# Weighing values by attention with the values stationary, in halves of the array, and raw scores in halves of its rows

## The chip, the core and the metric

One NeuronCore of a Trainium2 chip runs the whole program. The metric is the device time of one execution in microseconds; the kernel before and the kernel after are compared by the median of their runs. The engines have names in the profile: PE is TensorE's matmul, PEld its weight load, DVE is VectorE, ACT is ScalarE, POOL is GpSimd, SP issues the DMAs. They run side by side and meet only at semaphores.

## The reference

Attention over 2 batches, 8 heads, 768 positions and 64 values per head, with a mask: a query sees the first `n_sink` = 4 keys and the last `window` = 128 keys up to itself. Two feed-forward layers follow, on 1536 tokens of 512 values, 2048 hidden.

```
scores = q k^T / sqrt(64), masked;  a = softmax(scores);  x = a v
x = relu(x W_in)^2 W_out                                (layer 1)
h = x W2_in;  g = P(h) / (Q(h) + 1e-6);  out = g W2_out (layer 2)
P = a0 + a1 h + a2 h^2 + a3 h^3,  Q = 1 + |b0||h| + |b1| h^2
```

## The kernel before, in words

The time has three parts: a front in which only attention runs, layer 1, and layer 2. Layer 1 has four blocks of 384 tokens (3 tiles of 128) and 16 steps (`i`) a block. A step is 12 matmuls of `first1` (weights stationary, `xT` moving, 384 columns, into `h_ps`), the square on ACT and DVE (`relu`, `square`, `hidden`), and 12 of `second1` into `y_ps`. Both split each f32 operand into a rounded high part and a low part and make three products of type fp32r. The attention of later blocks is put between them: `events` gives a share to the middle of `first1` and to the middle of `second1` of each step, an order written out by hand and followed by every engine.

Attention has 96 units, one for each head of each query tile of 128. Unit u is tile `qt = u // 8`, head `m = u % 8`, and `i = qt % 6` is the tile's place in its batch. The units 0 to 29 (`LEAD = 30`) run in the front. Slot s does, in this order on PE: `score(s)`, `turn_p(s - 2)`, `weigh(s - 3)`.

- `score` (L1177): the keys of two tiles of 128 and, from `i = 2`, 32 columns with the sink keys, so 128, 256 or 288 columns. For the first 8 groups of four units (`EARLY = 8`) it is a raw f32 matmul (L1196) over 128 rows, of which the 64 lower ones hold zeros in q. Later k and q are split on POOL (`split_kq`, L475) and it is two fp32r matmuls (L1200). k and q are stored twice for that, in rows 0 to 63 and 64 to 127.
- DVE adds the mask and takes the row's greatest value in one instruction (`scores`, L918, output `bnegs`, a ring of 4).
- ACT makes the exponential and its sum (`exp`, L650). It writes `bprobs[:, r, cols, m % 4]`: the four heads of a group are interleaved, so a column of one head lies 16 bytes from the next.
- `turn_p` (L1204) transposes one or two tiles of it, and once for four heads the 32 x 4 sink columns of the group (L1218).
- DVE (even units) or ACT (odd units) copies the result to `bpT` (`pT_part`, L930 and L642).
- `weigh` (L1222): `bpT` (128 x 128) is stationary and 64 columns of `bv` move, so that the output has queries on the partitions (L1233). Once for four heads one product of the sinks with 256 moving columns (L1240) is added; `bvs` is zero outside the head's own block.
- When a tile's eight units are weighed, DVE sums and inverts the row sums and multiplies (`finish`, L938, into `o_sb`), PE turns `o_sb` by four transposes (`tile_out`, L1252), ACT writes the high part of `xT` (L672) and DVE the low part (L966).

POOL splits the weights (`weight_high` L456, `weight_low` L461), 8 tiles early (`EARLY_W = 8`), after which ACT makes the high parts and waits for the eighth at the end of step 0. SP issues all loads in order (`load_weights`, `load_k`, `load_q`, `load_v`, `load_sinks`), each behind a semaphore that frees its buffer.

PSUM has eight banks: four of `y_ps`, two of `s_ps`, `h_ps` and `o_ps`. In the front scores and transposes of odd units use banks of `y_ps`; in layer 1 there is one bank for scores and one for transposes.

## Time and profile before

| | us |
|---|---|
| median of 3 runs | 674.43 (673.2 to 674.54) |
| the profiled execution | 672.72 |
| its span, first to last instruction | 670.9 |
| PE busy | 654.5 (98%) |
| PEld busy | 617.3 (92%) |
| DVE busy | 447.9 (67%) |
| ACT busy | 377.7 (56%) |
| POOL busy | 330.9 (49%) |

Read these as averages over stages with different limits. Matmuls overlap one another, so that their durations add up to more than the time they take; the distance between starts is what one costs. A raw f32 matmul stands in the trace as two weight loads and two MATMULs.

### The profile page before, as it was taken

Reading aid. Unit: us, or ns where it says so; the run is one execution under the profiler, and the core shown is the slowest. Engines: PE = TensorE matmul, PEld = TensorE weight load, DVE = VectorE, ACT = ScalarE, POOL = GpSimd, SP = SyncE. Lnnn points to the kernel's source line nnn. Section 1 sums busy time; section 2 is a strip of 40 time slices with the busy share of each in tenths; the row PEclk is TensorE's granted clock in tenths of the full one; section 3 lists DMA queues with packets and bytes.
Section 4 is the critical chain, followed back from the end, with each engine's and each line's share of the span. In section 5 each row is a group of like instructions: output and inputs, shape, how many; then the busy total and the mean of one; then the engine's idle time right before and its main releaser. Section 6 shows DMA issues by size and latency. Waiting matters only on the chain.

```text
span 670.9 us, 10181 instructions
## 1 busy us (share of the span) xinstructions
PE 654.5 (98%) x3714; PEld 617.3 (92%) x3714; DVE 447.9 (67%) x665; ACT 377.7 (56%) x804; POOL 330.9 (49%) x316
## 2 busy tenths in 40 slices
PE   7999999999999999999999998999999999999997
PEld 6889998999999999999999997889899999999995
DVE  6656564444344344343466679999899989998995
ACT  3755555334444354443322256677877787778874
POOL 3968573313242212300022337777777767776773
PEclk9999999999999999999999999999999999999999
DMA  7743241203311113100043430002100210001001
GB/s 248 258 146 119 97 162 40 64 1 121 93 40 40 40 40 134 40 9 1 20 125 124 127 110 0 1 1 95 48 1 0 95 48 0 1 1 48 1 0 53
DMA packets 28971, 43.49 MB, mean 65 GB/s; under 512 B 4080, under 2 KB 19440, under 8 KB 28400
## 3 DMA queue, kind: packets, MB, share of 16 engines
q1 hardware_dynamic: 28912, 42.74, 19.6%
q8 instruction: 32, 0.52, 0.3%
q14 instruction: 27, 0.22, 0.1%
HBM read 36.44 MB, written 6.29 MB: 64 GB/s over the span
## 4 chain that ended last, share of the span: by engine, by line
PE 77%; DVE 14%; ACT 3%; issue 3%; POOL 2%; DMA 1%; DVEq 0%; SPq 0%; ACTq 0%; POOLq 0%
PE h_ps L1146 22%; PE y_ps L1158 18%; PE y_ps L1384 15%; PE s_ps L1146 7%; PE o_ps L1233 4%; PE o_ps L1146 3%; DVE s_ps L879 3%; PE s_ps L1216 2%; PE s_ps L1200 2%; DVE o_ps L879 2%; DVE sq L842 2%; DVE p_buf L882 1%; DVE p_buf L873 1%; DVE h_ps L879 1%; DMA y_scratch<-xT 1%
## 5 line engine op out<-in xcount | busy, mean ns | idle before, releaser
L1146 PE MATMUL h_ps<-xT,weights 128*128 128x384 f32 x960 | 190.2, 340 | 0.7 <-ACT sq L594 0.7
L1146 PEld LDWEIGHTS h_ps<-xT,weights 128*128 128x128 f32 x960 | 167.4, 188 | 2.5 <-issue 1.0
L1158 PE MATMUL y_ps<-hid,weights 128*128 128x384 f32 x768 | 156.7, 344 | 0.0
L1384 PE MATMUL y_ps<-weights,hid 128*128 128x512 f32 x576 | 144.3, 395 | 2.3 <-POOL hid L561 1.0
L1158 PEld LDWEIGHTS y_ps<-hid,weights 128*128 128x128 f32 x768 | 134.5, 188 | 0.7 <-issue 0.2
L1384 PEld LDWEIGHTS y_ps<-weights,hid 128*128 128x128 f32 x576 | 107.2, 188 | 24.3 <-POOL hid L561 2.4
L656 ACT ACTIVATE bprobs<-bnegs,neg_max 128x288 f32<-128x288 f32 (+2 forms) x96 | 72.0, 759 | 67.2 <-DVE neg_max L925 66.8
L842 DVE TENSOR_TENSOR sq<-sq 128x384 f32<-128x384 f32 x64 | 45.4, 710 | 88.9 <-ACT sq L594 88.8
L561 POOL TENSOR_TENSOR hid<-p_buf,hid 128x384 fp32r<-128x384 f32 x63 | 64.8, 1028 | 40.0 <-ACT hid L762 39.6
L552 POOL TENSOR_TENSOR q_buf<-h_abs,q_buf 128x384 f32<-128x384 f32 x64 | 64.8, 1013 | 34.5 <-ACT q_buf L617 32.0
L879 DVE RECIPROCAL s_ps<-q_buf 128x384 f32<-128x384 f32 x31 | 79.4, 2561 | 3.2
L848 DVE TENSOR_TENSOR hid<-sq,hid 128x384 fp32r<-128x384 f32 x64 | 53.4, 835 | 37.8 <-ACT hid L599 37.8
L482 POOL TENSOR_SCALAR bq_hi<-q_raw 128x512 fp32r<-128x512 f32 x16 | 10.7, 668 | 136.6 <-DMA q_raw<-in_q_pack 115.2
L458 POOL TENSOR_SCALAR weights<-weights_raw 128x1024 fp32r<-128x1024 f32 x24 | 26.2, 1092 | 104.3 <-DMA weights_raw<-in_w_pack 104.1
L594 ACT ACTIVATE sq<-h_ps 128x384 f32<-128x384 f32 x64 | 31.4, 491 | 74.6 <-PE h_ps L1146 74.6
L1146 PE MATMUL s_ps<-xT,weights 128*128 128x384 f32 x384 | 72.5, 337 | 0.0
L1146 PEld LDWEIGHTS s_ps<-xT,weights 128*128 128x128 f32 x384 | 68.3, 188 | 2.5
L556 POOL TENSOR_TENSOR p_buf<-p_buf,h_sb 128x384 f32<-128x384 f32 x64 | 65.3, 1020 | 0.0
L599 ACT ACTIVATE hid<-sq 128x384 fp32r<-128x384 f32 x64 | 33.6, 524 | 51.4 <-DVE sq L842 51.4
L925 DVE CUSTOM_DVE_ANT_0 bnegs<-s_ps,band_bias 128x288 f32<-128x288 f32 (+2 forms) x81 | 34.3, 423 | 36.2 <-PE s_ps L1200 30.3
L762 ACT ACTIVATE hid<-p_buf 128x384 fp32r<-128x384 f32 x63 | 33.0, 524 | 28.9 <-DVE p_buf L882 27.6
L617 ACT ACTIVATE q_buf<-h_abs,abs_b 128x384 f32<-128x384 f32 x64 | 45.4, 709 | 2.1
(102 smaller groups left out, 940.4 us busy)
## 6 DMA issues: line engine op xcount, KB each, us to landing
weights_raw<-in_w_pack SPq DMA_DIRECT2D x32, 512.0 KB, 4.6
bk_raw<-in_k_pack SPq DMA_DIRECT2D x24, 256.0 KB, 3.3
q_raw<-in_q_pack SPq DMA_DIRECT2D x24, 256.0 KB, 3.4
bv<-in_v_pack SPq DMA_DIRECT2D x24, 128.0 KB, 2.0
y_scratch<-xT SPq DMA_DIRECT2D x2, 1536.0 KB, 6.1
xT<-y_scratch SPq DMA_DIRECT2D x2, 1536.0 KB, 7.2
out_y<-out_stage SPq DMA_DIRECT2D x3, 768.0 KB, 3.5
out_y<-out_stage SPq DMA_DIRECT2D x3, 256.0 KB, 2.9
```

The lines of the kernel that those rows point to most:

```text
L552: pool.tensor_tensor(q_buf[:, i % RING, :], h_abs[:, i % RING, :], q_buf[:, i % RING, :], ALU.mult).then_inc(qmul_ready, 1)
L556: pool.tensor_tensor(p_buf[:, i % RING, :], p_buf[:, i % RING, :], h_sb[:, i % RING, :], ALU.mult).then_inc(pmul_ready, 1)
L561: pool.tensor_tensor(hid2[:, i % RING, LO, :], p_buf[:, i % RING, :], hid2[:, i % RING, HI, :].bitcast(F32), ALU.subtract).then_inc(hid_re ...
L617: nc.scalar.activation(q_buf[:, i % RING, :], h_abs[:, i % RING, :], ACT.Identity, scale=abs_b[:, 1:2], bias=abs_b[:, 0:1]).then_inc(lin_r ...
L656: nc.scalar.activation(bprobs[:, u // GROUP % 2, cols, m % GROUP], bnegs[:, u % N_RING, cols], ACT.Exp, scale=-1.0, bias=neg_max[:, m:m + ...
L842: nc.vector.tensor_tensor(sq[:, i % 2, :], sq[:, i % 2, :], sq[:, i % 2, :], ALU.mult).then_inc(act1_ready, 1)
L848: nc.vector.tensor_tensor(hid[:, i % 2, LO, :], sq[:, i % 2, :], hid[:, i % 2, HI, :].bitcast(F32), ALU.subtract).then_inc(hid_ready, 1)
L879: nc.vector.reciprocal(h_banks[r], q_buf[:, r, :]).then_inc(qinv_ready, 1)
L925: nc.vector.tensor_tensor_reduce(out=bnegs[:, u % N_RING, cols], in0=score_bank(u)[:, cols], in1=band_bias[:, kind, cols], scale=-SCALE, s ...
L1146: ins = nc.tensor.matmul(bank, weights[:, i, wp, W_IN, t * P:(t + 1) * P], x, start=(t == 0 and n == 0), stop=(t == KC - 1 and n == 2))
L1158: ins = nc.tensor.matmul(y_ps[:, m, 0:NT], weights[:, i, wp, W_OUT, m * P:(m + 1) * P], hid[:, i % 2, gp, :], start=(i == 0 and n == 0), s ...
L1384: ins = nc.tensor.matmul(y_bank(turn, t), hid2[:, i % RING, gp, t * P:(t + 1) * P], weights[:, i, wp, W_OUT, :], start=(i == 0 and n == 0) ...
```

## The change

Attention is regrouped. The unit of work is a pair of heads (`p`), 48 in all, and weighing takes four heads at once (`g`, 24 groups). 15 pairs run in the front, which are the same 30 heads and tiles. A step "A" scores pair p and, for odd p, weighs group (p - 3) / 2; a step "B" transposes pair p - 1; "F" turns the inverse sums; "M", "X" and "L" multiply and split the output.

- Weighing: `bv[:, t, 64 columns]` is stationary and 128 columns of `bpT` move. The output has the head's 64 values on partitions: the even head of a pair on 0 to 63, the odd one on 64 to 127. The sink product is made for each head. The output is born turned, so instead of it the inverse sums are spread over 512 columns (DVE), turned (PE, four transposes), copied (ACT), and multiplied (DVE).
- Raw scores: q and k of the two heads of a pair lie in rows 0 to 63 and 64 to 127, and each head's matmul uses its half of the rows. No zeros and no copy are loaded for them. k and q for the split scores are loaded apart (`load_kd`, `load_qd`), from group 6 and 8.
- `bprobs` has one row after the other for the heads, so that exp writes contiguously. DVE packs the sink columns of four heads into `bsinks` before they are transposed.
- Each pair's transposes go to two banks, of which DVE copies the first and ACT the second.
- The `bnegs` ring has 3 places, `bpT` holds two pairs; `EARLY_W` is 6.

```diff
-    LEAD = 30
+    P_ALL = PAIRS * TILES
+    LEAD = 15
+    EARLY_W = 6
     EARLY = 8
-    EARLY_W = 8
-    P_RING = 3
-    N_RING = 4
+    N_RING = 3
...
-        bprobs = sb("bprobs", [P, 2, BAND, GROUP], F32, band)
-        bpT = sb("bpT", [P, P_RING, 3 * P], F32, band)
+        bprobs = sb("bprobs", [P, 2, GROUP, BAND], F32, band)
+        bsinks = sb("bsinks", [P, 2, GROUP, SINK_CAP], F32, band)
+        bpT = sb("bpT", [P, (2 * GROUP + 1) * P], F32, band)
...
+        def steps(first, last):
+            found = []
+            for p in range(first, last):
+                qt = p // PAIRS - 1
+                found.append(("A", p))
+                if p % PAIRS == 1 and qt >= 0:
+                    found.append(("M", qt))
+                    found.append(("X", qt))
+                    if qt >= QT and qt % QT == QT - 1:
+                        found.append(("L", qt))
+                if p <= P_ALL:
+                    found.append(("B", p))
+                if p % PAIRS == 1 and qt >= 0 and not (qt >= QT and qt % QT == QT - 1):
+                    found.append(("L", qt))
+                if p % PAIRS == 0 and qt >= 0:
+                    found.append(("F", qt))
+            return found
...
+                for k in range(4, EARLY):
                     load_k(k)
                     load_q(k)
...
+                    load_weights(0, k)
+                    if k < EARLY - 2:
+                        load_kd(k + 2)
+                    if k == EARLY - 2:
+                        load_qd(EARLY)
+                    if k == EARLY - 1:
+                        load_kd(EARLY)
+                    load_v(k)
+                load_kd(EARLY + 1)
+                load_qd(EARLY + 1)
...
+                for i in range(EARLY_W - 2):
                     weight_high(0, i)
                     weight_low(i)
+                    if i == 1:
+                        split_sinks(0)
+                split_k(EARLY - 2)
+                split_k(EARLY - 1)
                 split_kq(EARLY)
+                for i in range(EARLY_W - 2, EARLY_W):
+                    weight_high(0, i)
+                    weight_low(i)
                 split_kq(EARLY + 1)
...
-                    nc.scalar.activation(bprobs[:, u // GROUP % 2, cols, m % GROUP], bnegs[:, u % N_RING, cols],
+                    nc.scalar.activation(bprobs[:, u // GROUP % 2, m % GROUP, cols], bnegs[:, u % N_RING, cols],
                                          ACT.Exp, scale=-1.0, bias=neg_max[:, m:m + 1],
...
+                def pack_sinks(g):
...
+                    nc.vector.tensor_copy(bsinks[:, g % 2, :, :], bprobs[:, g % 2, :, 0:SINK_CAP]
+                                          ).then_inc(sinks_packed, 1)
...
+                    nc.vector.tensor_copy(inv_rows[:, :, :], row_inv[:, :].rearrange("p (h o) -> p h o", o=1
+                                          ).to_broadcast([P, H, D])).then_inc(inv_spread, 1)
+
+                def divide(qt):
+
+                    dve.wait_ge(inv_copied, qt + 1)
+                    dve.wait_ge(g_pv, 2 * (qt + 1))
+                    nc.vector.tensor_tensor(inv_cols[:, :], o_ps[:, :], inv_cols[:, :], ALU.mult).then_inc(o_read, 1)
...
+                    for hp in range(2):
+                        if k < EARLY:
+                            rows = slice(D * hp, D * hp + D)
+                            ins = nc.tensor.matmul(pair_bank(p, hp)[:, cols],
+                                                   bq[rows, k % 3, P * (c % 2):P * (c % 2) + P], bk[rows, c, cols],
+                                                   start=True, stop=True)
+                            continue
...
+                def weigh(g):
+                    qt, c, i = pair(2 * g)
+                    wait_turned_copies(pe, 2 * g + 1)
+                    pe.wait_ge(bv_loaded[g % 4], 16 * (g // 4 + 1))
+                    if c == 0 and qt >= 1:
+                        pe.wait_ge(o_read, qt)
+                    last = c + 1 == KC - 1
+                    tiles = 1 if i == 0 else 2
+                    for t in range(tiles):
+                        for cc in (c, c + 1):
+                            for hp in range(2):
+                                at = D * (2 * cc + hp)
+                                ins = nc.tensor.matmul(o_ps[D * hp:D * hp + D, cc * P:(cc + 1) * P],
+                                                       bv[:, t, at:at + D], bpT[:, turned_at(cc, hp) + t * P:turned_at(cc, hp) + (t + 1) * P],
+                                                       start=(cc == 0 and t == 0),
+                                                       stop=(i < 2 and last and cc > c and t == tiles - 1),
+                                                       skip_group_check=True)
+                    if i >= 2:
...
+                                ins = nc.tensor.matmul(o_ps[D * hp:D * hp + D, cc * P:(cc + 1) * P],
+                                                       bvs[:, at:at + D], bpT[:, 2 * GROUP * P:(2 * GROUP + 1) * P], start=False,
+                                                       stop=(last and cc > c), skip_group_check=True)
```

## Rows read from the trace of the kernel before

**Rows 1.** The page: the span, and the first line of the engine totals.
```profile
span 670.9 us, 10181 instructions
...
PE 654.5 (98%) x3714; PEld 617.3 (92%) x3714; DVE 447.9 (67%) x665; ACT 377.7 (56%) x804; POOL 330.9 (49%) x316
```

**Rows 2.** Busy time by stretch (start:end, length, each engine), and a wait.
```profile
0.00:44.50 44.50, 39.21 (x237) 33.56 (x238) 28.39 (x107) 26.48 (x77) 27.59 (x26) 1.00 0.74 235
44.50:320.00 275.50, 271.14 (x1714) 267.13 (x1714) 127.60 (x303) 124.19 (x290) 92.30 (x80) 1.00 0.20 65
...
402.00:671.00 269.00, 262.18 (x1298) 234.62 (x1297) 240.64 (x198) 200.69 (x387) 191.37 (x192) 1.00 0.07 25
...
PE h_ps L1135 <- POOL ident L453: 2.0, 1, 2.0
```

**Rows 3.** Timeline of PE, one slot in layer 1: start, us, engine, line, operation.
```profile
190.68 1.21 PE L1146 MATMUL h_ps<-xT,weights 128*128 128x384 f32 x6
191.72 0.29 PE L1200 MATMUL s_ps<-bkT,bq_hi 128*128 128x288 f32 x1
...
191.99 0.39 PE L1216 MATMUL s_ps<-ident,bprobs 128*128 128x128 f32 x2
192.21 0.56 PE L1233 MATMUL o_ps<-bv,bpT 128*128 128x64 f32 x4
192.58 1.30 PE L1146 MATMUL h_ps<-xT,weights 128*128 128x384 f32 x6
193.72 1.22 PE L1158 MATMUL y_ps<-hid,weights 128*128 128x384 f32 x6
```

**Rows 4.** Timeline of PE in the front.
```profile
38.83 0.39 PE L1216 MATMUL s_ps<-ident,bprobs 128*128 128x128 f32 x2
39.05 0.56 PE L1233 MATMUL y_ps<-bv,bpT 128*128 128x64 f32 x4
39.45 0.65 PE L1240 MATMUL y_ps<-bvs,bpT 128*128 128x256 f32 x2
39.94 0.65 PE L1196 MATMUL y_ps<-bk_raw,q_raw 128*128 128x288 f32 x2
40.42 0.39 PE L1216 MATMUL y_ps<-ident,bprobs 128*128 128x128 f32 x2
```

**Rows 5.** Groups by line, 44.5 to 320 us (count | busy us, mean ns), and weight loads.
```profile
L1233 PE MATMUL o_ps<-bv,bpT 128*128 128x64 f32 x262 | 37.1, 261 | 0.3 <-DVE o_sb L949 0.3
...
L1240 PE MATMUL o_ps<-bvs,bpT 128*128 128x256 f32 x28 | 9.1, 407 | 0.0
...
L1146 PEld LDWEIGHTS h_ps<-xT,weights 128*128 128x128 f32 x960 | 167.4, 188 | 2.5 <-issue 1.0
```

**Rows 6.** Groups by line of ACT, over the whole span.
```profile
L656 ACT ACTIVATE bprobs<-bnegs,neg_max 128x288 f32<-128x288 f32 x64 | 52.1, 818 | 45.0 <-DVE neg_max L925 44.8
L617 ACT ACTIVATE q_buf<-h_abs,abs_b 128x384 f32<-128x384 f32 x64 | 45.4, 709 | 2.1
...
L647 ACT ACTIVATE bpT<-s_ps 128x256 f32<-128x256 f32 x17 | 6.5, 380 | 9.6 <-PE s_ps L1216 9.6
```

**Rows 7.** A group of DVE; timeline of POOL and DVE from 12 us.
```profile
L925 DVE CUSTOM_DVE_ANT_0 bnegs<-s_ps,band_bias 128x288 f32<-128x288 f32 x57 | 25.8, 453 | 26.9 <-PE s_ps L1200 23.4 <-PE s_ps L1196 3.5
...
12.08 2.36 POOL L463 TENSOR_TENSOR weights<-weights_raw,weights 128x1024 fp32r<-128x1024 f32 x1
...
12.71 1.77 DVE L889 TENSOR_SCALAR band_bias<-sq 128x32 bf16<-128x32 f32 x1
```

**Rows 8.** DMA issues (count, KB each, us to landing); timeline of POOL from 52 us.
```profile
weights_raw<-in_w_pack SPq DMA_DIRECT2D x32, 512.0 KB, 4.6
bk_raw<-in_k_pack SPq DMA_DIRECT2D x24, 256.0 KB, 3.3
...
53.19 2.57 POOL L463 TENSOR_TENSOR weights<-weights_raw,weights 128x1024 fp32r<-128x1024 f32 x1
```

563 lines of the change are left out of this document (287 added, 276 removed).

## The prediction

> **What bounds the kernel now.** I read the engine totals first, then busy time by stage. TensorE is busy 654.5 of 670.9 us, so the next question is where its rows differ [rows 1]. There are three stretches. Until 44.5 us lies the front: 30 of the 96 units of attention, with layer 1 not yet begun. TensorE is busy 39.2 of 44.5 us there, and 2.0 of the idle 5.3 us pass before its first instruction [rows 2]. From 44.5 to 320 us, layer 1 has the other units between its matmuls and TensorE is busy 271.1 of 275.5. What comes after 402 us is layer 2, which the change leaves alone. The granted clock is 1.00 in each [rows 2], so I give the clock no term. The bound is TensorE's instruction stream in the first 320 us; time that another engine saves there counts only where TensorE waits for it.
>
> So each piece of attention has to be priced in TensorE time, and a duration is the wrong price, since matmuls are pipelined. I take distances between starts. Six dense matmuls start at 190.68 and the next instruction at 191.72: 0.173 us each, though the six last 1.21, so that one lasts 0.34. Between the starts 190.68 and 193.72 lie twelve dense matmuls (2.08 us) and one unit, so a unit of 288 columns costs 0.96 us: two scores 0.27 (191.72 to 191.99), two transposes 0.22, and the rest, 0.47, for four weighing instructions, 0.115 each [rows 3]. In the front a raw score instruction of 288 columns costs 0.24 (39.94 to 40.42, two), a transpose 0.11 (38.83 to 39.05, two), a weighing instruction of 64 columns 0.10 (39.05 to 39.45, four), a sink instruction of 256 columns 0.245 [rows 4]. A raw f32 matmul is two instructions, as the counts of two show. A raw 128-column one should then stream 0.24 x 128/288 = 0.107 us; a 64-column one would need 0.053 but costs twice that, so its 128-column weight load sets its pace.
>
> **The change, part by part.**
>
> 1. Weighing in layer 1 (18 groups of four heads). Today: 262 instructions at 0.115 and 28 sink instructions [rows 5] at 0.24 x 256/288 = 0.21: 30.1 + 6.0 = 36.1 us. After: one matmul per head and key tile, two instructions, 64 stationary and 128 moving columns. 16 groups have two tiles (16 instructions), 2 have one (8), and 14 groups add 8 for the sinks, since each head now needs its own sink product: 272 + 112 = 384. One after the other at 0.11 they take 42.2 us, which is 6.1 more than now. If the two column halves work side by side, the order in the code (both instructions of one head, then both of the next) lets only the second of one head run with the first of the next: n instructions take n/2 + 1 places. That is 16 x 9 + 2 x 5 + 14 x 4 = 210 places; each needs 0.107 for the stream, and two loads of 64 columns, as much as the one load that costs 0.115 now: 24.2 us, a gain of 11.9. No row has two matmuls side by side, so the bounds are +6.1 and -11.9. I take the overlap because the halves share neither stationary columns nor output partitions, and a load already runs beside a dense matmul in every dense row.
>
> 2. Going over to halves and back. Two crossings per group of weighing, 36 in layer 1; in the front five per two pairs, 37 in all. No row shows one. From below: nothing, as the goings between raw and rounded matmuls at 191.99 and 192.58 leave the unit at the sum of its parts. From above: the last matmul must end (1.21 less 1.04 = 0.17 us [rows 3]) and the first load be made afresh (0.19 [rows 5]): 0.36. I take 0.15, nearest to the first of the two: the pipeline empties, the load is hidden. Layer 1: +5.4 us (0 to +13).
> The Trainium skill ("TensorEngine Tiling (Array Packing)", Tiling Modes) says that going to another tiling mode drains TensorE, and this speaks against the change; it gives no time. Without that rule the sum would be 8 us lower; with a drain at the upper bound, 13 us higher.
>
> 3. Raw scores in row halves, in the front: pairs 4 to 7 of 256 columns, 8 to 14 of 288. Four instructions per pair take three places: 4 x 0.21 + 7 x 0.24 = -2.5 us with overlap, 0 without. Weighing in the front, 27 units: 8 with one tile and 19 with two, 92 x 0.10, and 4 x 0.245 = 10.2 us now; after, 96 instructions, 54 places of 0.11 = 5.9 (10.6 without overlap): -4.3. Crossings 37 x 0.15 = 5.6, of which I count half, since TensorE idles 3.3 us there anyway and a wait also empties the pipeline: +2.8.
>
> 4. Exp in a row. Now 0.82 us for 288 columns. A contiguous ACTIVATE with pointers for scale and bias takes 0.71 for 384 [rows 6], so 288 lie between 0.53 (by columns alone) and 0.71; I take 0.63. 96 x 0.19 = up to 18 us of ACT, but ACT is busy 124 of 275 us in layer 1 [rows 2], so worth 0 there. In the front it shortens a chain that would be late next: with a pair's two exps (1.0 to 1.2) and a copy (0.38 for 256 columns [rows 6]), ACT needs 1.5 to 1.7 us a pair beside TensorE's 2.3. The stationary loads of the probabilities become contiguous too; a transpose already costs its stream, 0.11 against 0.107, so 0.
>
> 5. DVE gets more. Per pair: two reads of scores (0.45 each) [rows 7] and a copy (0.4, as ACT's [rows 6]), 1.3 us; per tile now also a spread of the inverses over 512 columns (like a product of 512 from SBUF, up to 0.7) beside the 0.7 us of multiplication and 0.7 of splitting, and per two pairs a packing of sinks (about 0.25): 1.3 + 2.1/4 + 0.12 = 1.9 us a pair. That fits under 2.3. But the spread and the packing read and write SBUF alone, and such operations of DVE are held while POOL runs: the bias of 32 columns that began at 12.71 ended at 14.48, with POOL's 12.08 + 2.36 = 14.44 [rows 7]. POOL is busy 27.6 of 44.5 us in the front and nearly always from 11 to 40. Three packings hold up the transposes of their pair directly. Six new operations at about half of a 2.4 us operation in the worst case give 0 to 7 us; I take +3 in the front, and +1 for the first block of layer 1.
> The Trainium skill ("SBUF — State Buffer", Who interferes with whom) calls this an exclusive lock that the later comer waits out in full; the row of the bias agrees.
>
> 6. Loads and POOL. Early k and q are no longer stored twice: of 256 KB each [rows 8] half goes, 8 x 256 KB less, but four doubled parts (kd 6 to 8, qd 8) come in their place, each with its issue on SP's in-order queue ahead of a v. A group then brings 1.15 MB per 4.6 us, 250 GB/s beside the 235 of now [rows 2]; they land in 3.3 to 4.6 us, and are asked for three pairs (7 us) ahead. POOL splits 6 weight tiles early, not 8, at 3.5 us each. Its eighth low part ends at 55.76 [rows 8] and ACT waits for it behind step 0. The sixth, moved behind the splits of k 6, 7 and group 8, would end near 47 to 50, before step 0 ends: -1. Cost if a load comes late: about 2 us, once.
>
> 7. The turned inverses take the place of the turned output: four transposes a tile either way, 0. One event now holds a pair's scores or its transposes, and dense work of 2.08 us lies between events; two score reads (0.85 us) fit. No term.
>
> **Sum.** Layer 1: -11.9 + 5.4 + 1 = -5.5. Front: -2.5 - 4.3 + 2.8 + 3 = -1.0. POOL -1. Together -7.5, against the profiled execution of 672.7 us (span 670.9 and 1.8 around it): 665.2. The median of the runs is 674.4, 1.7 higher; on that scale 666.9, said as 667.0.
>
> **The rivals.**
> - Crossings cost nothing and the front follows TensorE: 5.4 + 2.8 us off: 658.8. For it: the changes of data type cost nothing. Against: a half-array matmul is a different use of the array. 0.20.
> - The halves take turns (or a load of 64 columns costs what one of 128 does, which comes to the same): weighing +6.1 in place of -11.9 (18.0), the front loses 2.5 + 4.3 + 0.4 (7.2), and the crossings stand: 667.0 + 25.2 = 692.2; with free crossings 684. This ends slower. It decides, with the front left as forecast, at 36.1 - 5.4 - 1 + 1 + 1 = 31.7 us, 276 places of 0.115 for the 384 instructions of layer 1. For it: a raw f32 matmul holds its half for two instructions in a row, and no row shows any overlap. 0.22.
> - Overlap, but a crossing costs 0.36: 36 x 0.21 + 37 x 0.21 x 0.7 = 13 more: 680. 0.10.
> - The change does what it says but TensorE's savings are turned into waits, for DVE behind POOL in the front (its 7 us) and for unequal events in layer 1 (0.25 us at half of 33 pairs, 4): 667 + 8 = 675. 0.07.
> - The forecast, 667.0, itself 661.5 to 672.5: 0.41.
>
> **How the numbers follow.** The likeliest gives 667.0. The range must leave out no more than 0.2: 656 covers free crossings; above, 688 takes in the costly crossing and the free-crossing half of the second rival, and leaves out its worse half. A measurement here tells 0.2%, 1.3 us, from no change. Faster: nearly all of the forecast, the first rival and a part of the fourth: 0.61. Same: 0.07. Slower: 0.32.
>
> **What would show it.** In the profile after, weighing instructions of 128 moving columns that start in couples a few ns apart, nine places a group, or one every 0.11 us if not. The start of the first dense matmul behind a group, less 0.115 per place, is the crossing. The first dense matmul of layer 1 should start at 43 to 44 us; the 320 us mark move to about 312. Exps of 288 columns near 0.63 us; spreads or packings of over 1 us only beside POOL. I am wrong if couples are missing, if a crossing is above 0.25 us, or if TensorE's waits between 44 and 320 us grow beyond the 4.4 us of now.

## The result, and the profile after

The changed kernel takes 688.5 us (median; 686.2 to 690.3), the kernel before on the same chip 674.5: a ratio of 1.020, with a 95% interval of 1.015 to 1.025. I had forecast 667.0. It is slower, and it lies 0.5 us above the upper end of my range (656 to 688). The profiled execution took 687.67 us with a span of 685.8, against 672.7 and 670.9 before.

The page of the changed kernel first, as in [rows 1], then busy time by stretch, as in [rows 2] (start:end, length, then PE, PEld, DVE, ACT, POOL busy, the granted clock, DMA share, GB/s). The stretches are again the front, layer 1 with its attention, and the second layer:

```profile
span 685.8 us, 10452 instructions
...
PE 647.7 (94%) x3810; PEld 595.1 (87%) x3810; DVE 464.6 (68%) x693; ACT 369.7 (54%) x818; POOL 329.9 (48%) x312
```

```profile
0.00:53.70 53.70, 37.09 (x237) 24.08 (x238) 32.38 (x113) 25.08 (x82) 23.81 (x26) 0.84 0.54 171
53.70:343.50 289.80, 275.00 (x1856) 263.02 (x1857) 142.36 (x330) 119.53 (x300) 95.47 (x77) 0.98 0.19 61
417.00:685.80 268.80, 262.15 (x1298) 234.58 (x1296) 240.64 (x198) 200.86 (x387) 191.48 (x192) 1.00 0.07 25
```

TensorE has 6.8 us less to do and idles 38.1 us where it idled 16.4. In the front 16.6 of 53.7 us are idle (5.3 of 44.5 before), in layer 1 14.8 of 289.8. The second layer is as it was. So the saving is there, and the new idle time, 21.7 us, is more than three times as large. Not all of the loss is idle time: the granted clock, 1.00 in each stretch before, is 0.84 in the front now and 0.98 in layer 1.

For the place of the loss I use four marks from TensorE's timeline: where the first dense matmul of layer 1 starts, and where the last matmul of the second half of each block starts. Lengths of the stretches between them, in us:

| kernel | front | block 0 | block 1 | block 2 |
|---|---|---|---|---|
| before | 44.5 | 100.4 | 90.9 | 92.8 |
| changed | 53.7 | 103.6 | 90.9 | 95.3 |

So the front gives +9.2, block 0 +3.3, block 2 +2.5, block 1 nothing. The largest waits of TensorE, front and layer 1 (total, how often, the longest):

```profile
PE o_ps L1318 <- DVE bpT L1009: 4.1, 2, 3.1
PE y_ps L1341 <- DVE inv_rows L1022: 3.9, 3, 2.3
PE y_ps L1297 <- ACT bpT L716: 2.6, 4, 1.1
PE h_ps L1302 <- DVE bsinks L1001: 2.1, 3, 1.1
...
PE s_ps L1282 <- ACT bpT L716: 6.6, 2, 3.4
PE s_ps L1341 <- DVE bpT L1009: 4.8, 4, 2.9
PE s_ps L1297 <- DVE neg_max L989: 2.3, 4, 0.7
```

**The matmuls themselves came out better than forecast.** A group of four heads with two key tiles in layer 1, on TensorE's timeline (start, us, line, operation), to be read against [rows 3]:

```profile
193.69 0.28 PE L1282 MATMUL s_ps<-bkT,bq_hi 128*128 128x256 f32 x1
193.81 0.28 PE L1282 MATMUL s_ps<-bkT,bq_lo 128*128 128x256 f32 x1
194.01 1.09 PE L1318 MATMUL o_ps<-bpT,bv 128*64 128x128 f32 x16
195.04 1.16 PE L1221 MATMUL h_ps<-xT,weights 128*128 128x384 f32 x5
```

Sixteen instructions take 1.03 us from the first start to the start of the next dense matmul: nine places of 0.107 (0.96) and 0.07 for the way back. The way in is the 0.20 from the last score's start less the score's own 0.12: 0.08. So a crossing costs 0.07 to 0.08 us and not 0.15.

**One wait of 3.3 us in each of blocks 1 and 2.** Timelines of SP, ACT and TensorE of the changed kernel:

```profile
180.17 0.33 SPq L383 DMA_DIRECT2D bv<-in_v_pack  x1
180.55 0.43 SPq L399 DMA_DIRECT2D y_scratch<-xT  x1
...
186.74 0.63 ACT L730 ACTIVATE xT<-inv_cols 128x512 fp32r<-128x512 f32 x1 [3.66 <-DMA y_scratch<-xT]
187.28 0.49 ACT L707 ACTIVATE bprobs<-bnegs,neg_max 128x256 f32<-128x256 f32 x1
...
188.27 0.36 PE L1282 MATMUL s_ps<-bkT,bq_hi 128*128 128x256 f32 x1 [3.28 <-ACT bpT L716]
```

ACT's split of x for block 2 overwrites what `store_y(0)` saves, so it waits for that DMA. On SP's queue the store stands behind the load of v 15, which waits for a weighing to be done. In the kernel before the order on SP's queue is the same, and ACT waits for the store there too:

```profile
163.15 0.33 SPq L334 DMA_DIRECT2D bv<-in_v_pack  x1
163.94 0.35 SPq L347 DMA_DIRECT2D y_scratch<-xT  x1
...
170.09 0.60 ACT L672 ACTIVATE xT<-s_ps 128x512 fp32r<-128x512 f32 x1 [2.47 <-DMA y_scratch<-xT]
...
171.56 0.48 PE L1216 MATMUL s_ps<-ident,bprobs 128*128 128x128 f32 x2 [0.47 <-DVE xT L966]
```

The store is issued 16.6 us later in the changed kernel, but 12.4 of these only say that its block 1 begins later (at 157.3 and not 144.9). Within the block the store comes 4.2 us later and the split is ready for it 3.0 us later, so ACT's wait grows from 2.5 to 3.7 us (in block 2 from 2.0 to 3.7). What stands behind the wait counts for more. Before, that is the square; TensorE loses 0.47 us. Now exp and the copy of turned probabilities stand there, and TensorE waits 3.28 us for the copy.

**A wait also costs behind its end, in the clock.** After some long waits TensorE takes up its work at 1.2 GHz. The changed kernel has three such places in layer 1, at its start and after the waits that end at 103.8 and 282.8 us. Two of them (layout as above; the granted clock is the third number from the end):

```profile
104.00:109.00 5.00, 5.00 (x23) 5.00 (x22) 0.56 (x1) 1.96 (x3) 2.37 (x1) 0.66 0.02 3
281.00:289.00 8.00, 6.20 (x31) 6.20 (x32) 3.23 (x9) 3.96 (x11) 3.77 (x4) 0.79 0.13 47
```

The kernel before has 1.00 from end to end of these stretches. The price shows in block 1, where the same wait leaves the clock at 2.4 GHz in the changed kernel and at 1.2 in its first variant below (masks first). The six dense matmuls behind the wait, first in the changed kernel, then in the variant:

```profile
188.83 1.20 PE L1221 MATMUL h_ps<-xT,weights 128*128 128x384 f32 x6
...
186.33 0.55 PE L1281 MATMUL s_ps<-bkT,bq_hi 128*128 128x256 f32 x1 [3.25 <-ACT bpT L716]
187.32 2.12 PE L1220 MATMUL h_ps<-xT,weights 128*128 128x384 f32 x6
```

The block takes 90.9 us with the first and 92.7 with the second: 1.8 us for the clock alone.

**DVE held behind POOL.** One case in block 0 and one in the front (POOL and DVE timelines of the changed kernel):

```profile
100.57 2.34 POOL L529 TENSOR_TENSOR weights<-weights_raw,weights 128x1024 fp32r<-128x1024 f32 x1
100.92 2.28 DVE L1022 COPY inv_rows<-row_inv 128x512 f32<-128x512 f32 x1
103.12 0.41 DVE L1009 COPY bpT<-s_ps 128x256 f32<-128x256 f32 x1
103.79 0.63 PE L1341 MATMUL s_ps<-ident,inv_rows 128*128 128x128 f32 x4 [2.90 <-DVE bpT L1009]
...
10.74 2.34 POOL L529 TENSOR_TENSOR weights<-weights_raw,weights 128x1024 fp32r<-128x1024 f32 x1
10.86 2.44 DVE L952 TENSOR_SCALAR band_bias<-sq 128x128 bf16<-128x128 f32 x2
14.80 1.12 PE L1318 MATMUL o_ps<-bpT,bv 128*64 128x128 f32 x8 [3.09 <-DVE bpT L1009]
```

The spread of the inverses, whose median is 0.43 us, ends 0.3 us behind POOL's operation, and the bias 0.2 us behind its own, much as in [rows 7]. The first case is of the kind I had priced. The second is not new work at all: it is the bias of [rows 7], now in front of the copy that the first weighing needs.

### The profile page after: what moved, and what is told of

Its sections match the earlier page's. It is cut to its first block, busy times and chain, and to the rows that moved or that the text cites. A ratio compares the mean times of both kernels' runs of the same rounds, so it can differ in the third digit from the quotient of the medians.

```text
span 685.8 us, 10452 instructions
## 1 busy us (share of the span) xinstructions
PE 647.7 (94%) x3810; PEld 595.1 (87%) x3810; DVE 464.6 (68%) x693; ACT 369.7 (54%) x818; POOL 329.9 (48%) x312
## 4 chain that ended last, share of the span: by engine, by line
PE 75%; DVE 15%; issue 4%; ACT 2%; DMA 2%; POOL 2%; DVEq 0%; SPq 0%; ACTq 0%; POOLq 0%
PE h_ps L1221 22%; PE y_ps L1233 17%; PE y_ps L1468 15%; PE s_ps L1221 7%; PE o_ps L1318 4%; PE o_ps L1221 3%; DVE s_ps L942 3%; PE s_ps L1282 2%; DVE o_ps L942 2%; DMA y_scratch<-xT 2%; PE s_ps L1297 2%; DVE p_buf L945 1%; DVE p_buf L936 1%; DVE bnegs L989 1%; DVE h_ps L942 1%
## 5 line engine op out<-in xcount | busy, mean ns | idle before, releaser
L1221 PE MATMUL h_ps<-xT,weights 128*128 128x384 f32 x960 | 193.0, 344 | 1.3 <-ACT sq L653 0.7
L1221 PEld LDWEIGHTS h_ps<-xT,weights 128*128 128x128 f32 x960 | 171.0, 192 | 4.8 <-issue 1.7
L905 DVE TENSOR_TENSOR sq<-sq 128x384 f32<-128x384 f32 x64 | 37.3, 583 | 82.2 <-ACT sq L653 81.9
L707 ACT ACTIVATE bprobs<-bnegs,neg_max 128x288 f32<-128x288 f32 (+2 forms) x96 | 48.1, 502 | 75.0 <-DVE neg_max L989 74.9
L911 DVE TENSOR_TENSOR hid<-sq,hid 128x384 fp32r<-128x384 f32 x64 | 56.9, 890 | 37.8 <-ACT hid L658 37.8
L550 POOL TENSOR_SCALAR bq_hi<-qd_raw 128x512 fp32r<-128x512 f32 x16 | 11.2, 703 | 143.5 <-DMA qd_raw<-in_qd_pack 143.5
L524 POOL TENSOR_SCALAR weights<-weights_raw 128x1024 fp32r<-128x1024 f32 x22 | 23.6, 1070 | 101.3 <-DMA weights_raw<-in_w_pack 101.2
L989 DVE CUSTOM_DVE_ANT_0 bnegs<-s_ps,band_bias 128x288 f32<-128x288 f32 (+2 forms) x82 | 31.6, 422 | 23.5 <-PE s_ps L1282 21.8
```

The source lines that it names most:

```text
L707: nc.scalar.activation(bprobs[:, u // GROUP % 2, m % GROUP, cols], bnegs[:, u % N_RING, cols], ACT.Exp, scale=-1.0, bias=neg_max[:, m:m + ...
L905: nc.vector.tensor_tensor(sq[:, i % 2, :], sq[:, i % 2, :], sq[:, i % 2, :], ALU.mult).then_inc(act1_ready, 1)
L911: nc.vector.tensor_tensor(hid[:, i % 2, LO, :], sq[:, i % 2, :], hid[:, i % 2, HI, :].bitcast(F32), ALU.subtract).then_inc(hid_ready, 1)
L989: nc.vector.tensor_tensor_reduce(out=bnegs[:, u % N_RING, cols], in0=pair_bank(p, hp)[:, cols], in1=band_bias[:, kind, cols], scale=-SCALE ...
L1221: ins = nc.tensor.matmul(bank, weights[:, i, wp, W_IN, t * P:(t + 1) * P], x, start=(t == 0 and n == 0), stop=(t == KC - 1 and n == 2))
```

## The experiments

Ratios are to the kernel before on the same chip (it took 671.7 to 673.0 us there). Lengths of the stretches, as in the table above, are those of each profiled execution. Executions of one kernel differ: the twelve of T, the kernel with three edits, took 667.8 to 675.4 us, and the two slowest had the lowest granted clock (0.979, the two with the highest, 0.994, took 668.8). So a difference of 1 or 2 us in one stretch shows little by itself. Blocks 1 and 2 repeat best: in T and every variant of it they take 86.7 to 87.3 and 89.8 to 90.3 us.

| kernel | median | ratio (95%) | front | block 0 | block 1 | block 2 |
|---|---|---|---|---|---|---|
| masks first | 687.2 | 1.025 (1.020-1.029) | 49.1 | 105.7 | 92.7 | 95.4 |
| x behind copy | 688.1 | 1.025 (1.023-1.028) | 51.8 | 104.2 | 92.4 | 95.1 |
| stores early (S) | 677.4 | 1.008 (1.005-1.012) | 53.0 | 104.1 | 87.5 | 89.9 |
| copies on ACT | 683.3 | 1.019 (1.014-1.024) | 51.4 | 99.0 | 92.0 | 95.0 |
| three edits (T) | 670.2 | 0.997 (0.994-1.000) | 49.7 | 99.0 | 87.1 | 89.9 |
| T, fillers | 669.8 | 0.995 (0.992-0.998) | 49.9 | 99.1 | 86.7 | 89.9 |
| S, one half only | 701.7 | 1.044 (1.039-1.049) | 56.7 | 105.8 | 92.3 | 97.7 |
| S, strided exp | 678.4 | 1.008 (1.005-1.010) | 52.4 | 98.6 | 88.9 | 90.8 |
| T, inverses late | 675.7 | 1.004 (1.002-1.006) | 52.0 | 99.1 | 87.3 | 89.9 |
| S, full rows | 679.9 | 1.011 (1.008-1.013) | 56.1 | 100.7 | 87.2 | 89.9 |
| before, stores early | 671.9 | 0.998 (0.997-1.000) | 45.8 | 99.5 | 90.3 | 92.5 |
| T, weighing less | 667.5 | 0.992 (0.989-0.995) | 46.3 | 98.6 | 87.0 | 89.9 |
| T, short reads | 667.5 | 0.993 (0.990-0.995) | 49.2 | 99.7 | 87.2 | 89.9 |
| T, POOL's order | 671.8 | 0.999 (0.997-1.001) | 52.9 | 98.5 | 86.7 | 89.9 |
| T, finer events | 670.3 | 0.995 (0.993-0.998) | 50.8 | 98.5 | 87.0 | 89.8 |
| T, finer, fillers | 668.8 | 0.994 (0.991-0.997) | 49.1 | 99.8 | 86.7 | 89.8 |
| T, end of front | 668.7 | 0.994 (0.992-0.996) | 48.0 | 100.2 | 87.1 | 90.3 |
| all edits | 667.6 | 0.994 (0.991-0.996) | 49.0 | 97.7 | 87.1 | 89.8 |

**Masks first**

```diff
-                masks(0)
+                for n in range(4):
+                    masks(n)
                 for kind, n in steps(0, LEAD):
                     step(kind, n)
-                    if kind == "B" and n in (1, 2, 3):
-                        masks(n)
```

> The kernel after, with all four masks made by DVE ahead of the first scores, before POOL begins its weights. Theory: the front (first scores at 7.9 us, first dense matmul at 53.7) loses most of its 9.2 us because the second mask waits out POOL (2.4 us), TensorE then stands idle for 3.1 us and its clock is at half until about 26 us. Then the first dense matmul starts 5 to 8 us earlier and the time falls from 688.5 to about 681. Rival: the chain from a pair's scores through its exp and copy sets the pace of the front, and the clock falls anyway: 0 to 2 us.

The front is 4.6 us shorter, and the time is not: 687.2, a ratio that the interval does not tell from the changed kernel's. The theory on the time failed. That on the front came near: the start moved by 4.6 us where 5 to 8 were expected, so the rival's 0 to 2 us for the front failed too. The trace shows where the gain went in this execution. Block 0 is 2.0 us longer and block 1 1.8, and each has one more place where TensorE stands at 1.2 GHz behind a wait. The one in block 1 is shown above; the one in block 0 follows a wait of 1.15 us for a packing:

```profile
130.00:138.00 8.00, 7.27 (x41) 7.11 (x43) 3.14 (x10) 2.11 (x4) 0.59 (x1) 0.79 0.00 0
```

That the earlier start brings these two places about, and not the difference between executions, is not shown.

**x behind the copy**

```diff
-                    found.append(("X", qt))
+                    if qt >= QT:
+                        found.append(("X", qt))
...
+                if p % PAIRS == 1 and 0 <= qt < QT:
+                    found.append(("X", qt))
```

> The kernel after, with ACT's high part of the output (step X) behind the next exp and copy in the front, for the first three tiles. Theory: X waits for a weighing and a multiplication and holds up the exp behind it, and with it the transposes: three waits of TensorE of about 1.1 us go, 3 us together, 685. Rival: the transposes wait for the copy of the pair before in any case: 0 to 1 us.

The wait that it aimed at went from 2.6 us to 0.2 and the front became 1.9 us shorter, but the time did not fall, where 3 us were expected. Waits for the packing grew from 2.1 to 4.1 us, and block 1, with TensorE at 1.2 GHz behind the wait for the store, is 1.5 us longer.

**Stores early**

```diff
-                    if k == 15:
+                    if k == 14:
                         store_y(0)
-                    if k == 21:
+                    if k == 20:
                         store_y(1)
```

> The kernel after, with the two stores of layer 1's results issued one group earlier in SP's queue. Theory: ACT waits 3.7 us twice for the store (at 183 and 279 us), scores and dense matmuls behind it stand still, 3.3 and 3.4 us on TensorE and about 3.5 more with half a clock at 282: 6 to 9 us go, about 681. Rival: the wait moves to the loads behind the store in the same queue: 0 to 2 us.

The largest single cause: 688.5 becomes 677.4 (by the ratios, 1.020 becomes 1.008), and blocks 1 and 2 fall by 3.4 and 5.4 us. The waits were 3.3 and 3.4 of that; the other 2 us in block 2 are the clock, which is 1.00 there now (0.79 from 281 to 289 us before this edit). ACT's split no longer waits:

```profile
182.24 0.52 ACT L658 ACTIVATE hid<-sq 128x384 fp32r<-128x384 f32 x1 [0.62 <-DVE sq L905]
182.67 0.62 ACT L730 ACTIVATE xT<-inv_cols 128x512 fp32r<-128x512 f32 x1
183.19 0.49 ACT L707 ACTIVATE bprobs<-bnegs,neg_max 128x256 f32<-128x256 f32 x1
```

With that wait gone the two blocks show what the halves bring: 87.5 and 89.9 us against 90.9 and 92.8 before, 6.3 us for twelve groups.

**Copies on ACT.** `pack_sinks` and the spread of the inverses as ACT copies, the packing ahead of the pair's first exp, the spread behind it.

```diff
-                    nc.vector.tensor_copy(bsinks[:, g % 2, :, :], bprobs[:, g % 2, :, 0:SINK_CAP]
+                    nc.scalar.activation(bsinks[:, g % 2, :, :], bprobs[:, g % 2, :, 0:SINK_CAP], ACT.Copy
...
-                    nc.vector.tensor_copy(inv_rows[:, :, :], row_inv[:, :].rearrange("p (h o) -> p h o", o=1
-                                          ).to_broadcast([P, H, D])).then_inc(inv_spread, 1)
+                    nc.scalar.activation(inv_rows[:, :, :], row_inv[:, :].rearrange("p (h o) -> p h o", o=1
+                                         ).to_broadcast([P, H, D]), ACT.Copy).then_inc(inv_spread, 1)
```

> The kernel after, with the packing of the sinks and the spread of the inverses made by ACT, not by DVE. Theory: both are held on DVE while POOL runs, and TensorE waits 2.1 + 3.9 us for them in the front and about 5 in layer 1: 4 to 8 us go, 681 to 684. Rival: ACT is in the chain of exp and copy, and the 0.3 and 0.6 us that it takes on come back as waits: between -1 and +5 us.

Block 0 falls by 4.6 us and the front by 2.3; TensorE's waits ahead of the turning of the inverses between 60 and 340 us fall from 4.8 to 1.3 us. By the ratios alone (1.019 and 1.020) the gain is not told from nothing; that the copies and the masks count on top of the stores shows in the next run. The Trainium skill ("SBUF — State Buffer", Who interferes with whom) has the later comer of DVE and POOL wait the other out; the 2.28 us of a spread that takes 0.43 at the median agree. How much this costs depends on where POOL's operations happen to fall: the wait of 2.9 us at 103.8 is also absent from two runs below that leave the spread on DVE (strided exp, full rows), whose block 0 is 5.5 and 3.4 us shorter than that of S.

**Three edits together (T).**

> The changed kernel with three edits at once: y_scratch is stored one group earlier, the packing of the sinks and the spread of the inverses are copies of ACT and not of DVE, and all four masks are made ahead of the first pair. Theory (three separate waits stand in the way of what the halves save): the stores are worth 9 to 11 us, the copies 4 to 5, the masks 0 to 1 since the front hands its gain back to POOL's split weights and ACT's copies behind it: 672 to 675, that is level with the kernel before; the first dense matmul of layer 1 at about 48, block 0 of layer 1 in 99 to 100 us, blocks 1 and 2 in 88 and 90. Rival (the slack is one and the same, whatever frees it is spent at the next late load or split): 677, as with the stores alone.

The gains add up, and come to a little more than the 672 to 675 us expected: 670.2 us, 0.3% below the kernel before, at the edge of its interval. Blocks 0 to 2 are 1.4, 3.8 and 2.9 us shorter than before (8.1 together); the front is still 5.2 us longer. What is left of the question is the front.

**Fillers: what the clock costs.** T with 5, 2, 2 and 3 idle matmuls ahead of steps B 1 to 4.

```diff
+                    if kind == "B" and n in WARM:
+                        for w in range(WARM[n]):
+                            nc.tensor.matmul(y_ps[:, 3, 0:2 * P].rearrange("p (r n) -> p r n", r=2), ident[:, :],
```

> The last kernel with 5, 2, 2 and 3 filler matmuls (ident by twice ident, 256 columns, f32, into a bank of y_ps that is free then) ahead of the front's steps 1 to 4, where TensorE waits for masks and exp. It is to see what the half clock from about 13 to 25 us costs. Theory (the clock falls because TensorE idles there, and each microsecond at 0.50 costs half of one where TensorE is what is late): the granted clock stays at 1.00 to 28 us and the first dense matmul starts 1 to 4 us earlier. Rival (in the front ACT, DVE and POOL are late, not TensorE): the clock stays up but the first dense matmul moves by under 1 us, and the time by under 1 us.

Stretches 12 to 20 and 20 to 28 us of T, then of T with fillers; the granted clock is the third number from the end:

```profile
12.00:20.00 8.00, 5.43 (x26) 3.12 (x28) 3.27 (x13) 4.05 (x17) 6.58 (x6) 0.50 0.74 263
20.00:28.00 8.00, 6.62 (x52) 4.10 (x50) 4.78 (x17) 5.12 (x17) 6.95 (x5) 0.86 0.45 134
```

```profile
12.00:20.00 8.00, 6.89 (x48) 4.71 (x49) 3.49 (x14) 4.54 (x17) 6.81 (x7) 1.00 0.73 262
20.00:28.00 8.00, 5.76 (x51) 3.55 (x46) 5.64 (x22) 5.30 (x18) 7.83 (x5) 1.00 0.50 151
```

The clock stays at 2.4 GHz to 28 us and the front ends where it did (49.9 and 49.7). It is not at 2.4 GHz to the end: from 30 to 42 us it is 0.86 here and 1.00 in T. The medians differ by 0.4 us and the ratios, 0.997 and 0.995, are not told apart. So the rival holds as far as this goes: in this stretch, where TensorE waits for others, 1.2 GHz costs little. The intervals leave room for some 2 or 3 us, and it says nothing of layer 1, where TensorE is the bound.

**One half only: the overlap taken away.** Both heads of a pair go into columns 0 to 63 of the array, so their output lands on the same rows (left out of it: the second head's own place). With the stores early.

```diff
-                                ins = nc.tensor.matmul(o_ps[D * hp:D * hp + D, cc * P:(cc + 1) * P],
+                                ins = nc.tensor.matmul(o_ps[0:D, cc * P:(cc + 1) * P],
```

> With the stores one group earlier, both heads of a pair are weighed into the same half of the columns (output rows 0 to 63), so that no two matmuls can work side by side; instructions, loads, waits and the goings over to halves stay. The sums of two heads land on each other and are not the reference's. Theory (two matmuls in different column halves overlap, which is what the change gains): 384 places in layer 1 in place of 210 and 96 in place of 54 in the front, at 0.107: 18.6 + 4.5 = 23 us more than the kernel with the early stores (677.4), so 696 to 701; the weighing of a group with two key tiles takes 16 places of 0.11. Rival (there is no overlap, the halves take turns, and the weighing was cheap for another reason, as for its small loads): 676 to 680.

It costs 18 us by the spans of the profiled executions (694.8 and 676.6; the first is 5 us below its median) and 24 by the ratios; 23 were expected. The same group as above:

```profile
196.28 0.28 PE L1283 MATMUL s_ps<-bkT,bq_lo 128*128 128x256 f32 x1
196.49 1.96 PE L1319 MATMUL o_ps<-bpT,bv 128*64 128x128 f32 x16
198.38 1.33 PE L1222 MATMUL h_ps<-xT,weights 128*128 128x384 f32 x6
```

Sixteen instructions take 1.89 us in place of 1.03: 0.118 each, the way back included, one behind the other. So matmuls in the two column halves do run side by side, and the rival that the halves take turns is refuted.

**Strided exp**, with the stores early: `bprobs` as before, exp writing every fourth element, no packing.

```diff
-                    nc.scalar.activation(bprobs[:, u // GROUP % 2, m % GROUP, cols], bnegs[:, u % N_RING, cols],
+                    nc.scalar.activation(bprobs[:, u // GROUP % 2, cols, m % GROUP], bnegs[:, u % N_RING, cols],
```

> With the stores one group earlier, exp writes its probabilities strided over the four heads again, as in the kernel before, and the sinks are read in place, without the packing of DVE. Theory (ACT is no bound in layer 1, as I forecast, and the packing cost what it saved): the exps of 288 columns go back to 0.8 us, layer 1 stays within 1 us of the kernel with the early stores, the front loses 1 to 2 us by the longer exps and wins 1 to 2 by the packings: 676 to 679. Rival (each event holds a pair now, and the turning of the probabilities waits for ACT, so exp is on the path): 0.25 us at a good part of the 33 pairs and in the front: 681 to 686.

The medians, 678.4 and 677.4, are not told apart. The profiled execution is 3.1 us below its median, so its block 0, 5.5 us shorter, says little: what is gone there is the wait of 2.9 us for the spread, which this edit does not touch, and the 1.2 GHz behind it. Blocks 1 and 2, which repeat well elsewhere, are 1.4 and 0.9 longer, and the exps of 288 columns are back at 815 ns:

```profile
L707 ACT ACTIVATE bprobs<-bnegs,neg_max 128x288 f32<-128x288 f32 x64 | 50.7, 815 | 40.0 <-DVE neg_max L989 40.0
```

```profile
L707 ACT ACTIVATE bprobs<-bnegs,neg_max 128x288 f32<-128x288 f32 x64 | 33.8, 528 | 49.9 <-DVE neg_max L989 49.9
```

(first with the strided write, then the changed kernel). So the short exp is worth about 2.3 us for twelve groups in layer 1, where I had said nothing.

**Inverses late.** T with the turning of the inverses behind the next pair's scores and weighing, and division and split behind the next copies, in the front.

```diff
+                if p % PAIRS == 1 and 0 <= qt < QT:
+                    found.append(("F", qt))
...
+                if p % PAIRS == 1 and 0 <= qt < QT:
+                    found.append(("M", qt))
+                    found.append(("X", qt))
```

> The kernel with the three edits (stores, copies on ACT, masks first: 670.2), and besides in the front, for its three finished query tiles, the turning of the inverses comes after the next pair's scores and weighing and not before them, and the division and ACT's split of x come after the next copies and exps. Theory (in the front no engine is full; each tile puts a chain of sum, reciprocal, spread and turning, and then division and split, ahead of the scores, exps and copies that the next pair waits for, 1.1 to 2.2 us each on TensorE): two waits of 1.1 to 1.4 us a tile go, the first dense matmul of layer 1 starts at 44 to 46 in place of 49.7, and the time is 665 to 668. Rival (what is late is the chain of each pair itself, or POOL's splits of weights 4 and 5, which end at 55.8): the start moves by 1 to 2 us or the gain is given back in block 0, and the time is 669 to 671.

My theory fell, and the rival's 669 to 671 us too. The front grew by 2.3 us and the time by about 5. TensorE's waits for inverses are gone, and ahead of the weighing stand 4.2 us of waits for copies and 4.2 for which the profile shows no releaser (1.1 in T). It looks as if the turning had covered them. (Front, TensorE's waits.)

```profile
PE o_ps L1328 <- issue: 4.2, 4, 1.6
PE o_ps L1328 <- DVE bpT L1025: 4.2, 2, 2.7
PE h_ps L1231 <- ACT bpT L721: 2.9, 1, 2.9
```

**Full rows**, with the stores early: the raw scores contract over all 128 rows, so each head's scores are the sum of two heads'.

```diff
-                            rows = slice(D * hp, D * hp + D)
+                            rows = slice(0, P)
```

> The changed kernel with the stores one group earlier, and the front's raw scores contract over all 128 rows in place of a head's 64 (so both heads get the sum of the two heads' scores, which is not the reference's): no row halves are left, loads and instruction counts stay. Theory (the front is bound by its chain through DVE and ACT, so TensorE time saved there is worth little): the four score instructions of 288 columns take 0.96 in place of 0.69 us, the first dense matmul moves by under 1.5 us, 677 to 679. Rival (as I forecast: 2.5 us are saved there by the halves, all of them on the path): 679.5 to 681.

Four score instructions of 288 columns take 1.14 us in place of 0.76, first start to last end. The front is 3.1 us longer, more than my theory allowed and near the 2.5 of my forecast, but not all of it is the scores: from 36 to 46 us the granted clock is 0.83 here and 1.00 in S. Block 0 is 3.4 shorter, for the wait of 2.9 us behind POOL does not occur. The intervals of the ratios (1.011, 1.008) overlap. So score time in the front is on its path at least in part; how much the whole time feels of it is not shown.

**Before, stores early**: the control for the stores, the same edit in the kernel before.

> The kernel before with its stores one group earlier, a control. Theory (in the kernel before, the split of x did not wait for the stores, since the profile shows no such wait of TensorE): no change, 671 to 673. Rival (the stores stood in the way of both kernels and the 9 us are not the change's): 665 to 668.

0.2% (0.0 to 0.3). The 8 or 9 us of the stores belong to the change.

**Weighing less**: T, where the front's groups weigh one key tile and no sinks (that part of the output is left out).

```diff
-                    tiles = 1 if i == 0 else 2
+                    tiles = 1 if i == 0 or 2 * g + 1 < LEAD - 1 else 2
```

> The kernel with the three edits (670.2, first dense matmul of layer 1 at 49.7), and in the front the seven groups weigh one key tile and no sinks: that part of the output is left out. It takes about 2.5 to 3 us of TensorE's work away, 0.48 for each second tile and 0.44 for each group's sinks. Theory (the front is paced by each pair's chain, scores, DVE's read, exp, turning, copy, and the weighing lies beside it): the first dense matmul moves by under 1 us. Rival (TensorE's in-order work paces the front, as I forecast): it moves to 46.7 to 47.2.

The front is 3.5 us shorter, and the ratio is 0.992 against 0.997, with intervals that just overlap. The theory, under 1 us, does not hold, and the rival comes near: TensorE's work in the front counts, although TensorE idles a third of it (T's front: 34.0 of 49.7 us busy). Whether it counts in full is open, since the granted clock of the front is also higher, 0.93 against 0.90.

**Short reads**: T, where DVE reads 128 of the 256 or 288 score columns of pairs 4 to 14 (the rest of their scores is left out).

```diff
+                    if 4 <= p < LEAD:
+                        cols = slice(SINK_CAP + P * (i % 2), SINK_CAP + P * (i % 2) + P)
```

> The kernel with the three edits, and DVE reads only 128 of the 256 or 288 score columns of the front's pairs 4 to 14, so that the rest of their scores is left out; TensorE's and ACT's work are unchanged. Theory (the pair's chain paces the front, and both reads of a pair lie on it): 22 reads shorter by about 0.15 to 0.2 us each give 2.5 to 4.5 us, the first dense matmul at 45.5 to 47. Rival (TensorE's work or POOL's splits pace it): it moves by under 1 us.

Mixed. The time falls by 2.7 us, as the theory has it; the profiled execution (670.2) is the longest of this kernel and shows only 0.5 in the front. The ratios, 0.993 and 0.997, have overlapping intervals. I take from it, with the run above, that DVE's work and TensorE's both count, one behind the other and not beside each other; for DVE's this is likely, not shown.

**POOL's order**: T, all six weight tiles split in a row.

```diff
-                for i in range(EARLY_W - 2):
+                for i in range(EARLY_W):
```

> The kernel with the three edits, and POOL splits all six early weight tiles in a row, and k and q of the first groups of layer 1 behind them and not ahead of the last two. Theory (POOL is no bound of the front): 669.5 to 671.5, the same within 0.2%, the first dense matmul within 1 us of 49.7. Rival (the last two weight tiles, whose splits end at 55.8, hold ACT and DVE up in block 0): block 0 takes 97 to 98 us in place of 99.0, and the time is 668 to 669.

Not faster: 0.999 against 0.997, intervals overlapping. POOL's last two splits are not what is late. The front, 52.9, is 3.2 us longer in the profiled execution, beyond the 1 us expected.

**Finer events**: T, where DVE reads, TensorE turns and DVE copies the first head of a pair without waiting for the second.

```diff
-                    dve.wait_ge(p_scored, p + 1)
+                    dve.wait_ge(p_scored if hp else head_scored, p + 1)
...
-                    pe.wait_ge(u_exp, 2 * p + 2)
+                        pe.wait_ge(u_exp, 2 * p + 1 + hp)
```

> The kernel with the three edits (670.2, first dense matmul of layer 1 at 49.7), with a pair no longer handed over as one: DVE reads the first head's scores as soon as they are there, TensorE turns the first head's probabilities behind that head's exp, and DVE copies them behind those transposes. No work is added or taken away. Theory (a pair as one event puts TensorE, DVE and ACT one after the other): each hand-over comes 0.2 to 0.35 us earlier (half of the scores' 0.69, half of the transposes' 0.44) for the 15 pairs of the front: the first dense matmul at 43 to 47, and layer 1's waits of 4 us fall a little; 663 to 668. Rival (the front is paced by the second head's work, which comes no earlier, or by the order of the steps): it moves by under 1 us, 669.5 to 671.

No gain that can be told (670.3; front 50.8). That a pair is handed over as one is not the cause either: 663 to 668 us had been expected if it were. With the fillers besides:

> The same with the 5, 2, 2 and 3 filler matmuls ahead of the front's steps 1 to 4. Theory (the fillers lie in waits, and the half clock costs something once the hand-overs are shorter): 0 to 2 us below the last. Rival (they are work in a chain in which TensorE's work counts, 0.2 us each): 1 to 3 us above it.

668.8, not told from either.

**End of the front.** Where T's 5.2 us lie shows in the turnings at the ends of the three tiles. They start at 20.24, 30.82 and 41.04 in the kernel before and at 18.62, 30.26 and 41.79 in T. So T is 1.6 us ahead at the first, loses 2.4 in the two cycles that follow (in each TensorE waits 1.3 to 1.4 us for the inverses), and needs 7.9 us from the third to the first dense matmul, where the kernel before needs 3.5. (Not all of these 4.4 is loss: T has two pairs to transpose there, the kernel before two heads.) TensorE, DVE and ACT of T there:

```profile
45.10 0.76 PE L1281 MATMUL s_ps<-bk,bq 64*128 64x288 f32 x4
46.99 0.41 PE L1302 MATMUL y_ps<-ident,bprobs 128*128 128x128 f32 x2 [1.13 <-ACT bpT L716]
49.73 0.66 PE L1226 MATMUL h_ps<-xT,weights 128*128 128x384 f32 x1 [2.00 <-ACT bpT L716]
```

```profile
46.09 1.61 DVE L1042 TENSOR_TENSOR xT<-inv_cols,xT 128x512 fp32r<-128x512 f32 x1 [0.36 <-ACT xT L746]
```

```profile
48.11 0.54 ACT L707 ACTIVATE bprobs<-bnegs,neg_max 128x288 f32<-128x288 f32 x1 [1.06 <-DVE neg_max L1010]
...
49.16 0.47 ACT L716 ACTIVATE bpT<-h_ps 128x384 f32<-128x384 f32 x1
```

Two things that the change puts there. The low part of x is made from `inv_cols`, in SBUF, and is held behind POOL (1.61 us); the kernel before makes it from PSUM, and it takes 0.69:

```profile
42.60 0.69 DVE L966 TENSOR_TENSOR xT<-y_ps,xT 128x512 fp32r<-128x512 f32 x1 [1.34 <-ACT xT L672]
```

And pair 13 is turned into `h_ps`, the bank that layer 1's first matmul writes, so this matmul waits for ACT's copy, which stands behind pair 14's exps. The edit takes the second away: ACT copies first, and the first dense matmul waits for that copy alone.

```diff
-                wait_turned_copies(pe, LEAD - 2)
+                pe.wait_ge(pT_by_act, LEAD - 1)
                 first1(0, 0)
```

> The kernel with the three edits (670.2), and at the end of the front ACT copies pair 13's turned probabilities out of the h_ps bank ahead of pair 14's two exps, and the first dense matmul waits for that copy alone; for the copy out of y_ps the first matmul of the second half of layer 1 waits. Theory (the change turns probabilities into h_ps, so layer 1's first matmul, which writes that bank, waits for a copy that stands behind two exps; x_low, held behind POOL, ends at 47.7 and is next): the first dense matmul starts 1.2 to 1.7 us earlier, at 48.0 to 48.5, and the time falls by 1 to 1.7: 668.5 to 669.3. Rival (block 0 gives it back, since the exps and copies of pair 14 now come later): the start moves but the time stays within 0.5 us.

The first dense matmul starts at 48.0, as the theory has it. The median is 1.5 us lower, but block 0 of the profiled execution is 1.2 longer and its span the same as T's, and the intervals overlap; so part of it is shown, the start, and the gain in time is likely, not shown. The 1.2 us stand beside a lower clock: 0.72 from 48 to 60 us, 0.86 in T, and 1.00 in the kernel with all edits, whose block 0 is the shortest.

**All edits**

> All edits together: stores, copies on ACT, masks first, finer hand-overs, fillers, and the end of the front as in the last run. Theory (small gains add up): 667 to 668.5, a ratio to the kernel before of 0.992 to 0.994. Rival (the edits after the first three gain nothing that can be told): 669 to 670.5.

667.6 us, 0.65% below the kernel before (0.4 to 0.9%), the lowest of the kernels that compute the whole result, as the theory has it. Its interval overlaps T's (0.994 to 1.000), so that the edits after the first three gain anything is not shown. Against the changed kernel that is 2.7% by the ratios, with the same array work but for the fillers.

## Why the prediction was wrong

**Where it was right.** Step 1: the overlap is there, and nine places a group with two tiles is what the timeline shows (1.03 us); taking the overlap away costs what the sum says (24 us by the ratios, 23 expected). Step 2: a crossing costs 0.07 to 0.08 us, half of my 0.15. The Trainium skill ("TensorEngine Tiling (Array Packing)", Tiling Modes) says that the array is drained there; the rows bear that out as a gap, and show it to be short. With both, blocks 1 and 2 gain 6.3 us for twelve of eighteen groups once the stores are out of the way, where steps 1 and 2 give 6.5 for all eighteen, 4.3 for these. The short exp's 2.3 us (step 4 said 0) are about the difference. That the 4.3 fit is in part luck, for one reading in step 1 is wrong. Of the 0.47 us for four weighing instructions in [rows 3] only 0.37 lie ahead of the next dense matmul, 0.093 each; the other 0.10 is that the six dense matmuls behind them take 1.14 us (192.58 to 193.72) and not 1.04. The change does not remove such a return to dense work (its six dense matmuls behind a group, 195.04 to 196.21, take 1.17), it makes fewer of them: 51 in layer 1, one behind each turning and each weighing, where there were 66. So the gain of step 1 was over-sized and the cost of step 2 too. With 0.093 and 0.10, places of 0.107 and crossings of 0.075, I get 9.2 less 2.7, which is 6.5 again, an estimate from these rows.

**Step 6 failed, and cost most: 8 to 9 us.** Its worst case was a load that comes late, "about 2 us, once". I followed the loads that the change adds and moves, but not the stores that stand among them on SP's in-order queue, nor who waits for them. The change leaves their lines alone. The store now comes 4.2 to 4.7 us later in its block, and ACT's two waits for it grow from 4.5 to 7.4 us together; and exp and a copy, for which TensorE waits, have moved behind them, so that 6.6 us of them reach TensorE, and 2 us of clock come on top in block 2. In the kernel before such a wait reached it with 0.47 us. No row that I had shown has this; it takes SP's and ACT's timelines around the stores, with ACT's wait of 2.47 us: a wait that is there, and hurts hardly anybody yet.

**Step 5 was right in kind and too small.** Of spreads and packings behind POOL I took +3 in the front and +1 in block 0. Moving them to ACT gave 2.3 and 4.6; of the 4.6, 2.9 are one wait behind POOL, and the rest is about what the 1.2 GHz behind that wait costs. The rest of this term was outside my list: the biases, which DVE had to do before as well, now stand in front of the first weighing (4.6 us of the front, though the time did not fall by it alone).

**Step 7 failed.** "Four transposes a tile either way, 0" counts TensorE's instructions and not what they wait for. The inverses now make a chain of sum, reciprocal, spread and turning that ends in TensorE's queue (TensorE waits 3.9 us for it in the changed front, 5.0 in T), and x is split from SBUF and no longer from PSUM, so DVE can be held there too. That one event now holds a pair, for which I took no term, was no error by itself: finer events gained nothing that can be told.

**Step 3 sized the front by TensorE alone.** It counted what TensorE saves and half of the crossings. I left out that `h_ps` now holds probabilities at the front's end (1.7 us), and that TensorE's saving is not all that counts in a chain of engines: in T taking away work of TensorE's shortens the front, and taking away work of DVE's probably does. Of the 9.2 us the masks and the copies on ACT are 4.0 together (4.6 and 2.3, each by itself, would be 6.9: they cover each other), and the bank is 1.7. For the rest there are only T's rows: the waits for inverses of the last two tiles, 2.7, and the held split of x, 0.9, come to it, but no run removes them and keeps the gain. The run with the inverses late shows that the 2.7 cannot be had by moving them, and how much of them another order would save is left open.

**The clock.** "I give the clock no term" rested on the clock of the kernel before, and a change that adds waits can change the clock. In the front it fell to 0.84 and that cost little: the fillers, which brought it back from 12 to 28 us, gained 0.4 us at the median. In layer 1 it fell to 0.98, and there each place costs 1 to 2 us more than the wait ahead of it: with the late stores block 1 takes 90.9 us without one and 92.0, 92.4 or 92.7 with one, and one more in block 0 costs 2.0. Three places make 3 to 6 us of the changed kernel's time, an estimate from these pairs.

**The rivals.** The one that came nearest is the fourth, to which I gave 0.07 and 675: TensorE's savings turned into waits. Of its two parts DVE behind POOL held; unequal events are not borne out, since finer ones gained nothing that can be told. The stores and the clock were in no rival. Its price was 8 where 21 were lost; it would have taken a look at each step that ACT, DVE and SP do in order. The second rival, with 0.22, is refuted by the run with one half.

Of my own signs one told: I named TensorE's waits in layer 1 above 4.4 us as what would prove me wrong, and they are 14.8.

## What to carry to other kernels

When a change regroups work, list every wait of every in-order queue (DMA issues too) and ask when its releaser comes in the new grouping, even for lines that the diff does not touch. A wait that stops nobody in the profile before (2.47 us here) can stop everybody once other work stands behind it (3.28 us of TensorE). Price a moved engine step by the engine that runs beside it: a DVE operation with both ends in SBUF cost up to a whole POOL operation here (a spread 2.28 us and not 0.43, a split of x 1.61), the same work on ACT (0.63) or from PSUM (0.69) did not. Where the engine that waits is the bound, count the clock behind the wait as well. And when one wait is taken away, expect the next one behind it: alone, the first four edits gained 0 to 8 us by the ratios, and the two that shortened only the front gained nothing.

## What the runs showed of the hardware

- Two f32 matmuls with 64 stationary columns, in different column halves of the array, overlap: 16 instructions in 1.03 us, which is nine places of 0.107 and a crossing, against 1.89 in one half.
- Going from full width to column halves or back leaves a gap of 0.07 to 0.08 us.
- An exp that writes 288 elements in a row takes 0.53 us, one that writes every fourth 0.82. I had estimated 0.63.
- TensorE stood at 1.2 GHz from 12 to 20 us in T, behind 12 us of which it was busy 7.7, and a dozen idle matmuls kept it at 2.4 GHz to 28 us, which gained next to nothing.
- Behind the same wait of 3.3 us in layer 1 six dense matmuls took 1.20 us in one run and 2.12 in another: the same wait may or may not be followed by 1.2 GHz.
- A DVE copy of 512 columns within SBUF took 0.43 us at the median and 2.28 when it began behind a POOL operation.
